# Attention's last three tiles in a new order, logits by token, gates inverted per slot, and halved first loads

## The reference

```python
# attention: 4 batches, 8 heads, 768 positions, head size 64; 4 sink keys and a window of 128
scores = q @ k.T / 8
keep = (pos_k < 4) | ((rel >= 0) & (rel < 128))
scores = where(keep, scores, -1e9); scores -= max
a = exp(scores); a /= a.sum(-1) + 1e-9
x = a @ v                       # (3072 tokens, 512)
# mixture of experts: 8 experts, one for each token
logits = x @ w_gate; e = argmax(logits)
probs = exp(logits - logits.max()); probs /= probs.sum(-1) + 1e-9
y = probs[e] * (relu(x @ w1[e]) @ w2[e])       # 512 -> 1024 -> 512
# last stage
h = y @ w_in; out = (h - tanh(h)) @ w_out      # 512 -> 2048 -> 512
```

## Time and profile before

| what | us |
|---|---|
| median of 3 runs | 1114.25 |
| lowest, highest | 1113.52, 1114.8 |
| the profiled execution's own time | 1115.05 |
| its span, from the first to the last instruction | 1113.3 |
| attention, from 0 to the last scatter's issue | 186.55 |
| last scatter's issue to the first slot's first product | 10.25 |

### The profile page before, as it was taken

The page is one execution under the profiler, slowest core; times in us unless marked ns, Lnnn a source line. Parts: engine busy times, 40 slices in busy tenths (PEclk is TensorE's granted clock), DMA queues, the critical chain, the costliest instruction groups (busy, mean ns, idle before and its releaser), DMA issues.

```text
span 1113.3 us, 17138 instructions
## 1 busy us (share of the span) xinstructions
PE 1086.2 (98%) x6028; PEld 878.6 (79%) x6028; DVE 606.7 (54%) x1305; ACT 482.3 (43%) x1035; POOL 492.8 (44%) x496
## 2 busy tenths in 40 slices
PE   9999997999999999999989999999999999999995
PEld 6777875888888888888867888888888888888884
DVE  6787785223322232223268666666666666666664
ACT  7898884423241424442444333333333333333332
POOL 3266534707033517481374344335335335335332
PEclk9999999999999999999999999999999999999998
DMA  8636823525124444463232110001011011001000
GB/s 282 203 120 220 255 71 143 189 67 189 47 86 160 124 133 153 136 223 123 96 96 65 29 35 14 20 20 39 10 29 38 1 39 38 1 1 39 1 1 38
DMA packets 37917, 99.44 MB, mean 89 GB/s; under 512 B 8273, under 2 KB 8401, under 8 KB 32721
## 3 DMA queue, kind: packets, MB, share of 16 engines
q1 hardware_dynamic: 29392, 52.30, 15.2%
q0 software_dynamic: 8448, 46.17, 11.9%
HBM read 75.84 MB, written 22.61 MB: 88 GB/s over the span
## 4 chain that ended last, share of the span: by engine, by line
PE 92%; DVE 3%; POOL 2%; ACT 1%; issue 1%; DMA 1%; POOLq 0%; SPq 0%; DVEq 0%; ACTq 0%
PE bank L705 22%; PE bank L697 22%; PE bank L630 14%; PE bank L644 14%; PE bank L446 5%; PE bank L480 4%; PE bank L462 3%; PE bank L636 2%; PE bank L617 1%; PE bank L685 1%; PE bank L524 1%; POOL sq L1452 1%; PE bank L512 1%; PE bank L504 1%; DMA sorted_x<-x_tok,dest 0%
## 5 line engine op out<-in xcount | busy, mean ns | idle before, releaser
L1359 POOL TENSOR_TENSOR weights<-raw,weights 128x1024 fp32r<-128x1024 f32 x72 | 171.3, 2400 | 201.6 <-ACT weights L753 200.5
L697 PE MATMUL bank<-mT_hi,weights 128*128 128x512 f32 x768 | 251.9, 389 | 1.7 <-DVE mT_lo L1184 1.7
L705 PE MATMUL bank<-weights,gT_hi 128*128 128x512 f32 x768 | 241.9, 396 | 6.2 <-DVE gT_lo L1241 6.0
L1451 POOL TENSOR_SCALAR ser<-ser 128x512 f32<-128x512 f32 x96 | 63.9, 665 | 286.5 <-DVE ser L1223 286.3
L705 PEld LDWEIGHTS bank<-weights,gT_hi 128*128 128x128 f32 x768 | 142.1, 189 | 40.6 <-DVE gT_lo L1241 12.2
L697 PEld LDWEIGHTS bank<-mT_hi,weights 128*128 128x128 f32 x768 | 144.2, 188 | 31.8 <-DVE mT_lo L1184 2.0
L705 PE MATMUL bank<-weights,gT_lo 128*128 128x512 f32 x384 | 150.5, 392 | 0.0
L697 PE MATMUL bank<-mT_lo,weights 128*128 128x512 f32 x384 | 149.4, 389 | 0.0
L644 PE MATMUL bank<-weights,hT_hi 128*128 128x512 f32 x464 | 148.6, 401 | 0.0
L918 ACT ACTIVATE bank<-bank 128x512 f32<-128x512 f32 x96 | 55.9, 582 | 213.5 <-DVE ser L1233 213.5
L630 PE MATMUL bank<-weights,mT_hi 128*128 128x512 f32 x464 | 147.5, 399 | 0.0
(11 more groups left out here) (154 smaller groups left out, 1584.4 us busy)
## 6 DMA issues: line engine op xcount, KB each, us to landing
raw<-w_all POOLq DMA_DIRECT2D x32, 1024.0 KB, 5.5
raw<-w_all SPq DMA_DIRECT2D x8, 1024.0 KB, 7.6
sorted_y<-ys SPq DMA_DIRECT2D x30, 257.0 KB, 3.3
xs<-sorted_x SPq DMA_DIRECT2D x29, 257.0 KB, 2.8
kT<-kt SPq DMA_DIRECT2D x24, 264.0 KB, 3.1
qT<-qt SPq DMA_DIRECT2D x24, 256.0 KB, 3.9
v_in<-vt SPq DMA_DIRECT2D x24, 256.0 KB, 4.0
raw<-sorted_y SPq DMA_DIRECT2D x20, 257.0 KB, 2.7
```

What stands on the lines that cost most here:

```text
L697: done = e.matmul(bank[HB[n % 3]][:, :], wt[:, f // 2, c, cols], x[:, c, :], start=(c == 0 and m == 0), stop=(c == CH - 1 and m == 2))
L705: done = e.matmul(bank[YB[i]][:, :], x[:, n % 3, rows], wt[:, f, :], start=(f == 0 and m == 0), stop=(f == GCH - 1 and m == 2))
L1359: e.tensor_tensor(lo, src, hi.bitcast(F32), ALU.subtract).then_inc(s_w_lo, 1)
L1451: e.tensor_scalar(row, row, SERIES_2, 1.0, ALU.mult, ALU.add).then_inc(s_ser, 1)
```

## The change

- **First loads.** Tile 0's keys and queries come in halves of two head pairs; the queries' halves are issued by ACT. Tile 1's keys and queries are issued right behind, ahead of the values. `scores(0, 0)` waits for the first halves alone. The warm matmuls at the start are 5 instead of 8, and the 4 before the first transposes are gone.
- **Attention's end** is taken out of the loops and written out. On PE `rank(MULTI - 1)` stands behind the last tile's transposes, `sink_values` of tile 23 ahead of `turn_x(22)`, and `rank(MULTI + 1)` ahead of `turn_x(23)`. On DVE the set MULTI - 1's first `places` step stands ahead of `part(23, 2)`. On ACT `route_exp` of each set stands behind the `normalise` of the tile before.
- **Logits by token.** For tiles 22 and 23 the turned output is stationary and 16 columns of gate weights stream, so the result is token-major at once; `logits_evict` and `turn_logits` are gone for these, and `add_logits` takes over the sign.
- **Gates.** `gates` only sums; for the last three sets ACT's accumulator writes the sum straight into `x_tok`. 1e-9 and the reciprocal are done by DVE in every slot, on the column that `load_meta` brought; `finish` waits for that.
- **First slot.** It starts on the high part: eight products with `xT_hi`, then four with `xT_lo`. The transposes ahead of it are 5 instead of 11, the warm matmuls before 38 instead of 32.
- **SP** issues `clear_tail(1)` behind the first slot's load.

```diff
+            e.dma_start(kT[:, 0, 0:2, :].rearrange("p a n -> p (a n)"), kt[0, :, 0:2 * HALF]).then_inc(k_first, 16)
+            e.dma_start(kT[:, 0, 2:4, :].rearrange("p a n -> p (a n)"), kt[0, :, 2 * HALF:4 * HALF]).then_inc(k_in[0], 16)
+            load_keys(1)
+            load_queries(1)
...
             clear_tail(0)
-            clear_tail(1)
...
             load_x()
+            clear_tail(1)
...
-                    e.wait_ge(q_in[g % RING_Q], 16 * (g // RING_Q + 1))
-                    e.wait_ge(k_in[g % RING_K], 16 * (g // RING_K + 1))
+                    if g == 0:
+                        e.wait_ge(k_first, 16)
+                        e.wait_ge(q_first, 16)
+                    else:
+
+                        e.wait_ge(q_in[g % RING_Q], 16 * (g // RING_Q + (1 if g % RING_Q else 0)))
+                        e.wait_ge(k_in[g % RING_K], 16 * (g // RING_K + 1))
+                if pair == 2 and g == 0:
+                    e.wait_ge(k_in[0], 16)
+                    e.wait_ge(q_second, 16)
...
-                if p == 0 and g == 0:
-                    keep_warm(4, bk)
...
+            def logits_by_token(w):
+
+                e.wait_ge(s_oT, w + 1)
+                if w + 1 in sink_count:
+                    e.wait_ge(s_sinkT, sink_count[w + 1])
+                each = P // PAIRS
+                for c in range(PAIRS):
+                    at = R_TURNED.start + c * each
+                    done = e.matmul(logits_bank(w)[:, at:at + 2 * E], oT[:, w % 2, c, :], wg[:, c, 0:2 * E],
+                                    start=True, stop=True, skip_group_check=True)
+                done.then_inc(s_l_turned, 1)
...
-            keep_warm(8)
+            keep_warm(5)
...
-            keep_warm(32, bank[R_BANK])
+            keep_warm(38, bank[R_BANK])
...
+                def first_up():
+
+                    products = [(xT_hi, wt, c) for c in range(CH) for wt in (w1h, w1l)] + [(xT_lo, w1h, c) for c in range(CH)]
+                    for m, (xp, wt, c) in enumerate(products):
+                        if m < 2 * CH and m % 2 == 0:
+                            e.wait_ge(s_w_lo, c + 1)
+                        if m == 2 * CH:
+                            e.wait_ge(x_split, r["this"])
...
-                e.wait_ge(x_split, r["this"])
-                up(0, range(CH)).then_inc(h_first, 1)
+                if x == 0:
+                    e.wait_ge(x_hi, 1)
+                    first_up().then_inc(h_first, 1)
...
-            for _ in range(11):
+            for _ in range(5):
...
+            e.dma_start(qT[:, 0, 0:2, :].rearrange("p a n -> p (a n)"), qt[0, :, 0:2 * P]).then_inc(q_first, 16)
+            e.dma_start(qT[:, 0, 2:4, :].rearrange("p a n -> p (a n)"), qt[0, :, 2 * P:4 * P]).then_inc(q_second, 16)
...
+            part(ALL - 1, 3)
+            sinks_evict(ALL - 1)
+            route_exp(MULTI)
+            o_evict(ALL - 1)
+            normalise(ALL - 2)
+            route_exp(MULTI + 1)
+            normalise(ALL - 1)
+            route_exp(MULTI + 2)
...
+                e.tensor_reduce(x_tok[:, start % RING_X:start % RING_X + tiles, DM], expo[:, 0:tiles], AX_X,
+                                ALU.add).then_inc(s_gate, 1)
...
+                gate = ys[:, DM:DM + 1]
+                e.wait_ge(meta_in, r["this16"])
+                e.tensor_scalar(gate, gate, 1e-9, None, ALU.add).then_inc(gate_sum, 1)
+                e.wait_ge(gate_sum, r["this"])
+                e.reciprocal(gate, gate).then_inc(gate_done, 1)
```

More of the change, by code:

```diff
@@ L270, in norm_on_act, with first_of @@
             return w >= ALL - 2
+        def first_of(b):
+            return max(0, b - MULTI)
         def w_half(n, x):
@@ L592, in tensor @@
                     sink_values(g)
-                if i == ALL + 1:
-                    rank(MULTI + 1)
-                if 0 <= w < ALL:
+                if 0 <= w:
                     turn_logits(w)
[L597 to L600, removed]
+                turn_prob(i, 1)
+                if i - 3 in LAST and i < ALL - 1:
+                    rank(LAST.index(i - 3))
+            turn_prob(ALL - 1, 2)
+            turn_prob(ALL - 1, 3)
+            rank(MULTI - 1)
+            small_bank_read(ALL - 2)
+            turn_sinks(ALL - 1)
+            for p in range(PAIRS):
+                values(ALL - 1, p)
+            rank(MULTI)
+            logits_by_token(ALL - 2)
+            sink_values(ALL - 1)
+            turn_x(ALL - 2)
+            logits_by_token(ALL - 1)
+            rank(MULTI + 1)
+            turn_x(ALL - 1)
             keep_warm(5, bank[0])
@@ L646, in down @@
                     return done
-                e.wait_ge(x_split, r["this"])
-                up(0, range(CH)).then_inc(h_first, 1)
+                if x == 0:
+                    e.wait_ge(x_hi, 1)
+                    first_up().then_inc(h_first, 1)
+                else:
+                    e.wait_ge(x_split, r["this"])
+                    up(0, range(CH)).then_inc(h_first, 1)
                 up(1, range(0, 2))
@@ L847, in scalar @@
                     split_hi(0, i - 7)
-            r = {n: e.alloc_register(f"act_{n}") for n in ("this", "next", "this16", "trips")}
+            part(ALL - 1, 3)
[6 more added lines that the diff above has]
+            route_exp(MULTI + 2)
+            r = {n: e.alloc_register(f"act_{n}") for n in ("this", "next", "trips")}
             e.wait_ge(s_loops, 1)
@@ L867, in finish @@
                 e.wait_ge(y_done, r["this"])
[L868 removed]
+                e.wait_ge(gate_done, r["this"])
                 e.activation(ys[:, 0:DM], bank[MY][:, :], ACT.Copy, scale=ys[:, DM:DM + 1]).then_inc(y_copied, 1)
@@ L1029, in pick @@
                 hot = hot_all[:, start:start + tiles, :]
-                top, lg, sh, ky, rv = (x[:, 0:tiles] for x in (rmax, logit, shift, key, rev))
+                own = slice(first_of(b), first_of(b) + tiles)
+                top, lg, sh, ky, rv = (x[:, own] for x in (rmax, logit, shift, key, rev))
                 wide = top.unsqueeze(2).broadcast_to([P, tiles, E])
@@ L1141, in vector @@
                     sink_values_lo(i // TILES)
+            ranks_read = places(MULTI - 1)
+            next(ranks_read)
             part(ALL - 1, 2)
+            at_once(ranks_read)
             at_once(pick(MULTI))
-            at_once(places(MULTI - 1))
-            at_once(gates(MULTI))
+            invert(ALL - 2)
             at_once(places(MULTI))
-            invert(ALL - 2)
             add_logits(ALL - 2)
             at_once(pick(MULTI + 1))
-            at_once(gates(MULTI + 1))
             invert(ALL - 1)
@@ L1155, in vector @@
             at_once(pick(MULTI + 2))
-            at_once(gates(MULTI + 2))
             at_once(places(MULTI + 2))
@@ L1176, in vector @@
             e.tensor_copy(offs[:, :], sums[:, 1, 3:3 + E]).then_inc(s_offs, 1)
-            r = {n: e.alloc_register(f"dve_{n}") for n in ("this", "next", "trips")}
+            r = {n: e.alloc_register(f"dve_{n}") for n in ("this", "next", "this16", "trips")}
             e.reg_mov(r["this"], 1)
             e.reg_mov(r["next"], 2)
+            e.reg_mov(r["this16"], 16)
             def lower(out_, bk, hi):
@@ L1372, in scatter @@
                 e.wait_ge(s_dest, b + 1)
-                e.wait_ge(s_gate, b + 1)
+                if b < MULTI:
+                    e.wait_ge(s_gate, b + 1)
+                else:
+                    e.wait_ge(s_expo, b + 1)
                 e.wait_ge(s_ids, b + 1)
```

114 lines of the change are left out of this document (53 added, 61 removed).

## The result

| what | before | after |
|---|---|---|
| median of 5 runs, us | 1114.80 | 1109.98 |
| lowest, highest | 1113.52, 1115.57 | 1108.75, 1110.90 |
| the profiled execution's own time | 1115.05 | 1110.90 |
| its span | 1113.3 | 1109.1 |

The ratio is 0.9958, with a 95% interval of 0.9944 to 0.9973: faster, 4.8 us by the medians. The forecast was 1110.35 us. The time is right, in part by luck; the account behind it is right in the middle and wrong at the start, as the marks in the two traces show. A mark is an instruction that both kernels have; each number is its time after less its time before.

A forecast was written before the change was run, and what follows sets the result against it. PE was taken to bound the kernel, holding 92% of the last-ending chain. Terms 1.2 + 1.3 + 0.3 + 0.7 + 0.4 = 3.9 us, from 1114.25 to 1110.35; forecast's own range 1108.6 to 1112.0, with rivals 1108.2 to 1112.7.

The forecast's parts named there:

- The start: Tiles 0 and 1: earlier loads and fewer warm matmuls gain 1.2 us, between 0.3 and 1.5.
- I charge 0.3: At the start: 0.3 us deducted from the gain for PE running at the lower clock with fewer warm matmuls.
- PE is waited for little there: Tile 0 and part of tile 1: little waiting for PE even at 1.2 GHz, hence only 0.3 us charged.
- the first rival: Clock: slow start paces tile 1 by PE, one 1.6 us dip, first slot's dip stays; gain 1.9, 1112.35 us; chance 0.13.
- Up to the values: Attention's end, up to tile 23's values: `place` done sooner, so PE's wait before `turn_sinks` goes; gain 1.0 us, 0.5 to 1.0.
- From the values to the scatter: Attention's end, PE and ACT steps behind tile 23's values: last scatter issued 1.3 us earlier in all, range 0.6 to 1.8.
- the second rival: DVE's chain at attention's end later by 1 us, first halves no earlier than 4.2: gain 2.3, 1111.95 us; chance 0.11.
- The scatter: Last scatter, from issue to landing: 0.3 us shorter with one zero-row store moved behind the first slot's load; 0 to 0.8.
- The first slot: First slot after attention: starting on the high part alone, with low products last, gains 0.7 us.
- 0.4 for the clock: First 18 products of the first slot: half of 0.9 us of lower clock saved, between -0.4 and 0.9.
- The slots: DVE's two added one-column steps per slot, about 0.35 us: cost 0 while the column lands before about 224.7 us.
- the fourth rival: DVE's in-order wait for `meta_in` lengthens each of 29 slots; with 0.3 us late, 1119.05 us, slower; chance 0.04.

The follow-up runs named there:

- s_warm12: Changed kernel with all twelve warm matmuls of the start back (8, and 4 before the first transposes), halved loads kept: 1116.90 us, ratio 0.9986.
- b_warm6: Changed kernel with 6 instead of 5 warm matmuls at the start and the 4 before the first transposes back: 1110.25 us, ratio 0.9959.
- t_clear: Changed kernel with `clear_tail(1)` issued ahead of the first slot's load again: 1110.23 us, ratio 0.9957.
- t_first: Changed kernel with the first slot waiting for the low part again, behind 11 transposes: 1110.73 us, ratio 0.9961.
- t_warm32: Changed kernel with 32 instead of 38 warm matmuls behind attention: 1111.42 us, ratio 0.9963.
- a_after: The changed kernel, unedited, run again on the second chip: 1109.76 us, ratio 0.9964 to the kernel before.
- g_scalar: Changed kernel with DVE's addition of 1e-9 put back behind the gates, its result unread: 1116.31 us beside 1118.19 for the kernel before.

## Why the prediction was right, and where it was not

**The start was wrong.** The step that failed is "I charge 0.3" for the lower clock. The loads came as taken (scores at 3.75 for 3.6, bounds 3.2 to 4.2). But the low clock then lay on PE's path: the first four score products took 0.83 us instead of 0.48, the first exponential came at 5.03 where 4.6 was forecast, tile 1's scores took 2.06 us and DVE and ACT waited for them. "PE is waited for little there" was read from a start at full speed. Instead of 1.2 us gained, 0.68 was lost. This is the first half of the first rival, priced there at 1.6 us; it cost 1.9. Over the nine kernels whose start is the changed one (five warm matmuls), tile 0's values follow the clock: they came at 10.07 where it was up at 4.63, at 10.94 to 11.20 with the clock up between 8.71 and 9.61, and at 11.46 to 12.17 with it up between 10.18 and 11.35. With nine to twelve warm matmuls it was up early in three of five (4.30, 4.32, 4.39; 10.03, 10.52). The Trainium skill ("TensorE: Matmul & The Clock Gate", part 1) says that activity releases the clock. One in nine against three in five points that way, but s_warm12 and b_warm6 were as busy and stayed low, so the number of warm matmuls doesn't settle it. The term's size over these nine is between +0.9 and -1.2 us against the 11.00 of one trace, and negative in six.

**Up to the values** the forecast was 1.0, measured 0.86. The new order is 0.53 of it; the rest is argued to be the two steps of `gates`, which the forecast had put into that same wait.

**From the values to the scatter** 0.3 was forecast (1.3 less the 1.0), measured 0.65. The logits by token cost 1.04 us (in the chain 0.90) where 0.8 was taken, inside the bounds; ACT's chain behind `o_evict` shrank by 0.66, from 4.52 to 3.86, where 0.2 was taken: its short instructions overlap their neighbours, and the waits ahead of them are gone. Not all of that reached the scatter, because DVE, whose end behind the values stayed where it was, is now the later one by 0.17. The forecast had said that both end together and that a later DVE would take some back; the second rival's full 1 us wasn't met.

**The scatter** gave nothing of its 0.3. It lasts between 4.25 and 5.03 us over these kernels, and t_clear has one of the shorter ones with the store back.

**The first slot.** 0.7 forecast for the high part, 0.78 shown. 0.4 for the clock, 1.05 measured: the whole dip went, and half was charged. Neither the 38 warm matmuls nor the 5 transposes are shown to be the reason. The first product started at 192.82, near the 193.3 that the prediction names; its "about 4.5 us earlier than 196.8" doesn't fit that number, since its own terms give 3.9 less 0.4, or 3.5, and measured was 3.98.

**The slots** cost nothing, as forecast; the fourth rival is refuted by 357.92 against 357.96 us.

**What wasn't forecast.** 0.73 at tile 8, from the addition in `gates` (0.47 shown) and, it would seem, its neighbour. There the prediction's "The steps that leave `gates` lie in DVE time that waits for scores" failed. 1.62 at tile 13, a dip at 103.28 that the trace of before has and that of after lacks; t_first to t_warm32 and a_after lack it too. And 0.8 lost in the last stage, where the trace of after has one dip more (windows: length, PE busy, granted clock, DMA share):

```profile
1092.60:1096.00 3.40, 3.39 (x8) 0.50 0.00 0
```

So of 4.2 us between the profiled executions, 0.73 + 0.86 + 0.65 + 0.78 = 3.0 is work and waiting taken away, and 1.62 + 1.05 - 0.8 - 0.68 = 1.2 is the start and the clock, now up and now down. The sum 3.9 came out right by luck: the start's miss of 1.9 and the scatter's of 0.3 were made good by the tile 8 gain (0.73) and the first slot's clock (0.65 more than charged), and in this pair of traces by the dip at tile 13 (1.62 less the 0.8 of the last stage). No kernel tried here beats the changed one: b_warm6 has 0.9959 and a_after 0.9964, with intervals that overlap almost wholly.

## What to carry to other kernels

Read a term at the start of a program with TensorE's clock at both levels: what PE does "in the shade" at 2.4 GHz may be the path at 1.2. Before forecasting an edit that removes a small instruction, look at the longest of its kind, not at the median: one of seven additions took 1.35 us instead of 0.17, behind another engine, and 0.47 us of that lay on the path. And judge steps of under 1 us by marks in the traces of both kernels; the ratio of whole times can't tell them, and clock dips of 1.6 us come and go between executions.

## What the runs showed of the hardware

- A DVE addition of one constant to 128x6 float32, SBUF to SBUF, that starts beside a running GpSimd product ends with it (1.35 us in the kernel before, 1.47 and 1.46 in g_scalar; 0.17 where no product runs beside it); a reciprocal of that size and the sum of `gates` beside the same product don't wait (0.18 and 0.19). The cast of 128x8 counts to bfloat16 (`seen_b`), which the changed kernel keeps, does: 0.67 us at 60.72, ending with a GpSimd instruction of 0.73, and 0.17 for the one at 170.04 with none beside it.
- In 14 traces TensorE's full clock is first granted between 4.30 and 4.63 us (4 of them) or between 8.71 and 11.35 (10), and identical instruction streams at the start are in both groups. Later dips to 1.2 GHz last about 3.4 us (three near attention's end on the first chip 6.8) and come at various places.
- Four products with 16 moving columns and 128-column stationaries in float32 (eight instructions in the trace) take 1.04 us, four with 128 moving columns and 32-column stationaries 0.42. Their weight loads keep PEld busy for 0.97 and 0.16 us: with so few moving columns the loads of the stationaries set the time.
- On one chip ACT waited 1.0 us at one place and started 2.4 to 3.1 us late at another, in all four kernels, for nothing that the profile names; in none of the other traces.
